# Attention and two feed-forward blocks on one core: a third set of head operands, a second output place, another order of the paired work

## What is computed

```python
# 4 batches, 8 heads, 576 positions, head size 64
scores = (q @ k.T) / 8;  bias = -(cum[i] - cum[j]),  cum = cumsum(max(s, 0))
attn = softmax(where(causal, -1e9, scores + min(bias, 0)))
x = (attn @ v), heads side by side                      # 4 x 576 x 512
h = max(x @ w_in, 0)                                    # 1024 wide
conv = 3 taps along the positions, per channel
x1 = (h * sigmoid(conv)) @ w_out                        # 512 wide
u = x1 + (x1.T @ U @ V).T                               # rank 32, over positions
out = u + max(u @ w_ch1, 0) @ w_ch2                     # 2048 wide
```

## Time and profile before

| | us |
|---|---|
| median of 3 runs | 910.75 (907.56 to 912.88) |
| the profiled execution | 910.62 |
| its span, first to last instruction | 908.8 |
| PE busy in it | 861.6 |
| DVE busy, ACT busy | 468.5, 372.5 |

### The profile page before, as it was taken

The page is one execution under the profiler, slowest core; times in us unless marked ns, Lnnn a source line. Parts: engine busy times, 40 slices in busy tenths (PEclk is TensorE's granted clock), DMA queues, the critical chain, the costliest instruction groups (busy, mean ns, idle before and its releaser), DMA issues.

```text
span 908.8 us, 15655 instructions
## 1 busy us (share of the span) xinstructions
PE 861.6 (95%) x6184; PEld 809.2 (89%) x6184; DVE 468.5 (52%) x984; ACT 372.5 (41%) x709; POOL 50.6 (6%) x105
## 2 busy tenths in 40 slices
PE   4888898989999999999999999999999999999998
PEld 3666888879998999889998999988999999999998
DVE  6788694464445934555344871455323761442222
ACT  2777675554425634544332653444221431221110
POOL 3021000000000000000000000000000000000000
PEclk9999998989999999999999999999999999999999
DMA  7686945636663557336545454435444444274441
GB/s 162 164 228 157 305 141 189 222 73 199 214 209 104 188 167 259 127 106 212 180 152 177 129 172 145 134 100 184 146 145 169 141 174 150 94 240 182 150 175 53
DMA packets 64396, 150.36 MB, mean 165 GB/s; under 512 B 30026, under 2 KB 44362, under 8 KB 51780
## 3 DMA queue, kind: packets, MB, share of 16 engines
q1 hardware_dynamic: 61252, 144.50, 49.4%
q0 software_dynamic: 3072, 4.87, 2.1%
HBM read 119.15 MB, written 30.11 MB: 164 GB/s over the span
## 4 chain that ended last, share of the span: by engine, by line
PE 66%; DVE 13%; issue 10%; ACT 5%; DMA 4%; POOL 1%; SPq 1%; DVEq 0%; ACTq 0%; POOLq 0%
PE psum L1190 18%; PE psum L1192 18%; PE psum L1191 17%; PE psum L1169 5%; DVE work L958 2%; DVE psum L899 2%; PE psum L1116 2%; DVE work L961 2%; DMA few_scratch<-few 2%; PE psum L1148 2%; PE psum L1146 2%; DMA spread_out<-few_scratch 2%; DVE work L956 1%; ACT work L746 1%; DVE ybuf L973 1%
## 5 line engine op out<-in xcount | busy, mean ns | idle before, releaser
L1190 PE MATMUL psum<-r_hl,ring 128*128 128x288 f32 x512 | 153.6, 300 | 3.2 <-DVE r_hl L1001 1.7
L1190 PE MATMUL psum<-uu_hl,ring 128*128 128x288 f32 x512 | 153.2, 299 | 1.5 <-DVE r_hl L1001 1.5
L1192 PE MATMUL psum<-r_hl,ring 128*128 128x288 f32 x512 | 151.2, 295 | 0.0
L1191 PE MATMUL psum<-r_hl,ring 128*128 128x288 f32 x512 | 151.1, 295 | 0.0
L1192 PE MATMUL psum<-uu_hl,ring 128*128 128x288 f32 x512 | 151.0, 295 | 0.0
L1191 PE MATMUL psum<-uu_hl,ring 128*128 128x288 f32 x512 | 150.9, 295 | 0.0
L783 ACT ACTIVATE r_hl<-psum 128x288 fp32r<-128x288 f32 x128 | 52.5, 411 | 188.1 <-PE psum L1192 188.0
L1001 DVE SCALAR_TENSOR_TENSOR r_hl<-psum,r_hl 128x288 fp32r<-128x288 f32 x128 | 58.5, 458 | 134.7 <-ACT r_hl L783 134.6
L1169 PE MATMUL psum<-probs,va 128*65 128x320 f32 (+4 forms) x448 | 109.6, 364 | 6.5 <-ACT probs L694 6.3
L899 DVE CUSTOM_DVE_ANT_0 psum<-psum,key_late 128x512 f32<-128x512 f32 (+4 forms) x160 | 84.9, 564 | 57.1 <-PE psum L1116 56.8
L1190 PEld LDWEIGHTS psum<-r_hl,ring 128*128 128x128 f32 x512 | 96.6, 189 | 5.5 <-DVE u_acc L1013 2.7
(11 more groups left out here) (101 smaller groups left out, 1626.6 us busy)
## 6 DMA issues: line engine op xcount, KB each, us to landing
ring<-w_scratch SPq DMA_DIRECT2D x74, 1024.0 KB, 4.9
w_scratch<-ring SPq DMA_DIRECT2D x24, 1024.0 KB, 6.1
kq_raw<-in_kq_t SPq DMA_DIRECT2D x64, 288.0 KB, 5.0
stage<-in_w_ch SPq DMA_DIRECT2D x16, 512.0 KB, 4.7
spread_out<-few_scratch POOLq DMA_DIRECT2D x32, 144.0 KB, 3.2
out_t<-u_acc SPq DMA_DIRECT2D x16, 288.0 KB, 3.7
va<-in_v SPq DMA_DIRECT2D x32, 128.0 KB, 2.8
stage<-in_w_out SPq DMA_DIRECT2D x4, 512.0 KB, 6.5
```

Of the source, the lines that this page charges most:

```text
L1190: pe.matmul(o, hi, m_hi, start=start, stop=False)
L1191: pe.matmul(o, hi, m_lo, start=False, stop=False)
L1192: return pe.matmul(o, lo, m_hi, start=False, stop=stop)
```

## The change

1. **Third operands.** In body 0, `kb`, `qb`, `qc` get a third buffer (in `r_hl[0]`, not yet in use); the preparation of head n waits for head n-3 and moves from g 3 to g 1 (h < 6), DVE's copies and low parts to g 2. POOL sets one more region to ones.
2. **Two output places.** Heads of batch 0 write by turns to `O0` and `O0 + 4 * BANK`; in body 0 their eviction follows the next head's first exponentials.
3. The weight block's high and low part of body 0 move to g 3; the splits of x pairs 0 and 1 of batch 0 move into the first step of body 1.
4. At (1, 3) the transpose of the maxima moves from g 3 to g 4.
5. In `order`, late pairs stand elsewhere: none between the `gated` items, two behind `wo`, two ahead of `rank`, none behind `split`.
6. `first_products`: at the first `wi`, `wo` and `up` both halves of all tiles but the last are multiplied before the wait for the last tile. `rank` takes the turned tiles in their order and waits for each.
7. In bodies 1 to 3 the low parts of heads come one step later; the eviction follows the step's items where these hold turn, rank or mix; the last inversion of a batch comes at (7, 4) instead of in the next body; other steps for normalisation and splits.
8. For batch 3 the middle tap is on ACT.

```diff
+        def nth_pair(n):
+            return n % 3 if n < H else n % 2
+        def pair_before(n):
+            return max(n - 3, -2) if n < H else n - 2
+        kb, qb, qc = kb + [r_hl[0][:, 0, :]], qb + [r_hl[0][:, 1, :]], qc + [r_hl[0][0:KROWS, 2, :]]
+        def out_at(n):
+            return O0 + 4 * BANK * (n < H and n % 2 == 0)
+        def turn_at(a, h):
+            return TURN[a > 0] + ((a, h) == (1, 3))
             fill(1)
-            seq.append(("gated", b, 0, FT - 1, 0))
-            fill(1)
-            seq.append(("gated", b, 0, FT - 1, 1))
+            seq.extend(pair("gated", b, FT - 1))
             for d in range(KT):
                 seq.extend(pair("wo", b, d))
-            fill(1)
+            fill(2)
...
-                fill(1)
+                fill(2)
                 seq.extend(pair("rank", b, 0))
...
                 seq.append(("split", b, 0, KT - 1, 0))
-                fill(1)
...
-        X_SPLIT = [{(5, 0): 0, (7, 0): 1}, {(4, 0): 0, (6, 0): 1}]
-        X_SPLIT_LAST = [{}, {(0, 2): (NPAIR - 2,), (1, 0): (NPAIR - 1,)}, {(0, 0): (NPAIR - 2,), (0, 2): (NPAIR - 1,)}]
-        NORMALISE = [(4, 6), (3, 5, 7)]
+        EVICT_LATE = {(a, h) for a in PLAN for h in range(H - 1)
+                      if any(x[0] in ("turn", "rank", "mix") for x in PLAN[a][GROUPS * h + GROUPS - 1])}
+        X_SPLIT = {(5, 0): 0, (7, 0): 1}
+        X_SPLIT_LAST = [{}, {(0, 0): (0, 1), (0, 3): (NPAIR - 2,), (1, 0): (NPAIR - 1,)}, {(0, 0): (NPAIR - 2,), (0, 2): (NPAIR - 1,)}]
+        NORMALISE = [{(4, 2): 0, (6, 2): 1}, {(4, 1): 0, (6, 1): 1, (7, 3): 2}]
...
+                pool.memset(qc[2][D:KROWS - 1, :].bitcast(F32), 1.0).then_inc(s_rows1, 1)
...
                 def attention_step(a, h, g):                       # ScalarE
-                    if g == TURN[a > 0]:
+                    if g == turn_at(a, h):
                         max_to_row(a, h + 1)
-                    if g == 3 and not a:
-                        prepare_keys(a, h + 2)
-                        prepare_queries(a, h + 2)
-                    if g == 4:
+                    if g == 4 and (a or h == H - 1) and (a, h) not in EVICT_LATE:
                         evict_head(a, h)
                     for c in {0: (0, 1), 1: (2,), 2: (3,)}.get(g, ()):
                         exponentials(a, h, c)
+                    if g == 0 and h and not a:
+                        evict_head(a, h - 1)
+                    if g == (1 if h < H - 2 else 3) and not a:
+                        prepare_keys(a, h + 2)
+                        prepare_queries(a, h + 2)
...
+                def middle_tap(b, f):
+                    m = b * FT + f
+                    relu.wait(act, b, 2 * f + 2)
+                    yl_done.wait(act, m - 2)
+                    act.activation(conv[f % 2], hid[:, f % 2, 1:S + 1], ACT.Copy, scale=cw[:, 1, f:f + 1]).then_inc(cv.sem, 1)
...
-                    if g == 1 and h in WEIGHTS_HEADS:
+                    if g == 3 and h in WEIGHTS_HEADS:
                         weights_high(MADE[WEIGHTS_HEADS.index(h)])
...
                 def then(a, h, g):                                 # VectorE
-                    if g == 3 and not a:
+                    if g == (2 if h < H - 2 else 3) and not a:
                         highs(a, h + 2)
                         key_low(a, h + 2)
                         query_low(a, h + 2)
-                    if g == 3 and h in (2, 4, 6):
+                    if g == 4 - (a > 0) and h in (2, 4, 6):
                         invert_few(a, h // 2 - 1)
-                    if g == 2 and a:
+                    if g == 3 and a:
                         key_low(a, h + 2)
-                    if g == 3 and a:
+                    if g == 4 and a:
                         query_low(a, h + 2)
+                    if a and (h, g) == (H - 1, 4):
+                        invert_few(a, NPAIR - 1)
...
-                        evict.wait(pe, n - 1)
+                        evict.wait(pe, max(n - 2, -1) if n < H else n - 1)
...
+                def first_products(item, tiles, m_hi, m_lo, ready):
+                    if item[-1] == 0:
+                        other = (*item[:-1], 1)
+                        products(item, tiles, m_hi, m_lo, ready, range(tiles - 1))
+                        if BEFORE[other]:
+                            evicted(BEFORE[other])
+                        products(other, tiles, m_hi, m_lo, None, range(tiles - 1))
+                    return products(item, tiles, m_hi, m_lo, ready, range(tiles - 1, tiles))
```

More of the change, by code:

```diff
@@ L814, in ffn_step @@
                         hidden(b, i, half)
+                        if half and b == B - 1:
+                            middle_tap(b, i)
                         if i and not half:
@@ L926, in then @@
                 def then(a, h, g):
-                    if not a and g == 2 and (h, 0) in X_SPLIT[0]:
-                        x_low(a, X_SPLIT[0][h, 0])
-                    if a and (h, g) in X_SPLIT[1]:
-                        x_low(a, X_SPLIT[1][h, g])
-                    if g == 3 and not a:
+                    if g == (2 if h < H - 2 else 3) and not a:
                         highs(a, h + 2)
@@ L1215, in evicted, with products @@
                         acc.wait(pe, b, NTH[item] + 1)
-                def products(item, tiles, m_hi, m_lo, ready=None):
+                def products(item, tiles, m_hi, m_lo, ready=None, ks=None):
                     half = item[-1]
                     hi, lo = weights(item)
-                    for k in range(tiles):
+                    for k in ks or range(tiles):
                         if ready:
@@ L1230, in wi @@
                     x_ready = lambda k: xl_done.wait(pe, b * NPAIR + k)
-                    products(item, KT, *x_hl, x_ready if f == 0 and half == 0 else None).then_inc(mm_wi.sem, 1)
+                    (products(item, KT, *x_hl) if f else first_products(item, KT, *x_hl, x_ready)).then_inc(mm_wi.sem, 1)
                 def wo(item):
@@ L1235, in wo @@
                     y_ready = lambda k: yl_done.wait(pe, b * FT + k)
-                    products(item, FT, *y_hl, y_ready if d == 0 and half == 0 else None).then_inc(mm_wo.sem, 1)
+                    (products(item, FT, *y_hl) if d else first_products(item, FT, *y_hl, y_ready)).then_inc(mm_wo.sem, 1)
                 def turn(b, t, half):
@@ L1248, in rank @@
                 def rank(b, half):
-                    x1l.wait(pe, b)
                     w = DM // 2
-                    for t in range(NT):
-                        u = [x[:, t, :] for x in u_hl]
-                        m = [x[:, t, half * w:(half + 1) * w] for x in x1t_hl]
-                        mm = three(bank_at("rank", b, 0, 0, half)[:, 0:w], u[0], u[1], m[0], m[1], t == 0, t == NT - 1)
+                    parts = {}
+                    for x in SEQ:
+                        if x[:2] == ("turn", b) and (x[3] < NT - 1 or x[4] == half):
+                            parts[x[3]] = NTH[x] + 1
+                    for x, t in enumerate(sorted(parts, key=parts.get)):
+                        x1l.wait(pe, b, parts[t])
+                        u = [y[:, t, :] for y in u_hl]
+                        m = [y[:, t, half * w:(half + 1) * w] for y in x1t_hl]
+                        mm = three(bank_at("rank", b, 0, 0, half)[:, 0:w], u[0], u[1], m[0], m[1], x == 0, x == NT - 1)
                     mm.then_inc(mm_g.sem, 1)
@@ L1266, in up @@
                     u_ready = lambda k: ul.wait(pe, b, k + 1)
-                    products(item, KT, *uu_hl, u_ready if unit == 0 and f == 0 and half == 0 else None).then_inc(mm_up.sem, 1)
+                    (products(item, KT, *uu_hl) if unit or f else first_products(item, KT, *uu_hl, u_ready)).then_inc(mm_up.sem, 1)
                 def down(item):
```

71 lines of the change are left out of this document (41 added, 30 removed).

## The result

| | before | after |
|---|---|---|
| median | 910.06 us (906.86 to 914.1, 8 runs) | 902.03 us (899.29 to 907.1, 8 runs) |
| ratio | | 0.9912 [0.9883, 0.9942] |
| profiled execution's span | 908.8 us | 901.5 us |

Faster by 0.9%: 8.0 us where 20.0 were forecast, and 2 us above the upper end of the range.

The account below looks back on a forecast made before the run. PE, busy 95% of the span, was taken to be held by VectorE or ScalarE, not weight DMAs. Terms A to G sum to 20.0 us, with 1.7 of hidden waits given back: 910.7 - 20.0 = 890.7, said as 891, range 883 to 900.

Parts of the forecast that it names:

- Term A: Head loop of batch 0 up to the first w_in: shorter PE waits per head, 3.6 us gained, bounds 0 and 7.5.
- the rival of the shared engines: Row sums' spread comes later on the shared DMA engines, 2.0 us at the first w_in: 893, chance 0.08.
- its new wait sets the clock to half: First stage gives nothing, or a new wait at heads 7 and 8 of batch 0 halves the clock: 894.6 to 898, chance 0.17.
- B: Batch 1, head 3, transpose moved to g 4: wait 2.9 and half clock 3.0 go, 5.9 us; bounds 2.4 and 6.3.
- C: Turning, rank and mix of batch 0: waits of 1.50 and 1.20 us go, 2.7 us; bounds 1.2 to 4.
- the fourth rival: Edits move waits instead of removing them, half of terms C to G lost: 896 to 901, chance 0.08.
- The second half-clock stretch: After the mix wait of batch 0; kept in the forecast, costs up to 3.3 us; its going: about 888, chance 0.22.
- D: Batches 1 to 3, waits for x_low before the first w_in: nearly all go, 3.9 us.
- E: Batches 1 to 3, up products' r_hl waits: evictions go behind the items, 1.5 of 3.3 us.
- F: Batches 1 to 3, two r_hl waits of 0.86 at a down soon after its up: both go, 1.7 us.
- G: u_acc wait before batch 3's w_out goes, 0.7 us; the other u_acc waits stay.
- The signs that were named: Batch 0 heads 6.3 to 7.1 us apart, waits gone, PE idle near 30; wrong if new waits over 2 us or half-clock stretches.

Follow-up runs that it names:

- without early blocks: Changed kernel with the two w_out blocks no longer made early in batch 0 but in batch 1: 898.50 us, ratio 0.9897.
- The kernel with the late small load: Kernel before, with the third copy of the taps, U and V loaded at head 5 instead of head 2 of batch 0: 911.89 us, ratio 1.0028.
- without the early stores: Changed kernel without the two 1 MB stores in the stage of batch 0, w_out blocks then holding other numbers: 896.23 us, ratio 0.9871.
- the old loop without early blocks: Changed kernel with no w_out block made early and the head loop of batch 0 as before: 898.88 us, ratio 0.9906.
- The fillers: Idle matmuls ahead of PE's waits in heads 4 to 7 of batch 0, on the changed kernel with small load and store later, three operand pairs to head 11: 900.46 us.

## Why the prediction was wrong

**Term A failed, and with it the number.** "What bounds the stage" was read from the engines: a head of 7.97 us less two waits. The step that failed is "a head free of them is 7.97 - 1.6 = 6.4 us ... 6.8 to 6.9 us a head". It holds for the first heads (6.9 to 7.0 us from mark 2 to mark 4). It leaves out that a faster loop asks sooner for transfers that do not come sooner: the strip of v took 7.9 us to land in the kernel before and 9.6 in the changed one, and the 1.8 us that the old loop had to spare for it became a wait of 3.10. The earlier trace rows had the DMA share at 0.75 over the stage; over 48 to 54 us it was 0.98 in the kernel before, a window that I did not look at. I had the rival of the shared engines, but for the row sums' way before w_in alone, at 2.0 us and a chance of 0.08; in two kernels that way held the maxima inside the stage. The Trainium skill's rule quoted there (page "Trainium Kernel Development and Optimization", Key Constraints, that all queues' transfers share the 16 engines and interleave) agrees with this trace as far as it can show it: POOL's spreads of the row sums landed in a median of 5.3 us between 36 and 64 us, beside SP's loads and stores, and in 3.2 over the whole span. What the runs give for the loop in place of the forecast gain: 5.5 us lost in the profiled stage, 2.7 in the mean of four profiles of the same code, 4.8 in medians with the loop alone on the kernel before, and 2.2 with the rest of the change, which is not clear of noise. (The sum of A also takes the 0.2 us of an inversion off four heads, where the inversions at g 4 of heads 2 and 4 stand ahead of two of them; that is 0.4 us.)

**The other half of A is the clock.** The rival "its new wait sets the clock to half" (0.17, 894.6 to 898) names heads 7 and 8. In the profiled execution half clock came two heads sooner, behind the wait for v, and once more there, so both rivals happened in part, together. The prediction let each cause stand alone. It counted what waits are removed, never what their removal does to the granted clock elsewhere. The runs show that this is of the same size: new loop 5.2 us fewer waits, 4.6 more lost to the clock without early blocks; 0.7 and 5.3 on the kernel before.

**B** was right in place and sized 5.9; it measured 4.8, and 4.6 alone. The wait went; the next late thing, y_low, shows no wait. Of 6.8 us at half clock all went at that place, but in the one kernel with the transpose back only 3.4 had come. The kernel with the late small load had the same 2.87 us wait and no stretch behind it, with marks 12 to 13 at 35.14: the wait alone is 2.1, where the forecast had 2.9 for it, and the 6.8 us at half clock are the other 2.7.

**C** said 2.7 and measured 1.5. Rank's wait went. Mix's went only in name: where one of 1.20 us ended at 195.41, PE now stands for the exponentials (timelines of PE, the changed kernel and the one with no late eviction):

```profile
195.80 1.28 PE L1210 MATMUL psum<-probs,va 128*65 128x320 f32 x2 [1.59 <-ACT probs L717]
...
195.25 1.33 PE L1210 MATMUL psum<-probs,va 128*65 128x320 f32 x2 [1.58 <-ACT probs L717]
```

ScalarE is not ready sooner there in any of the three: an eviction stands ahead of these exponentials, which start at 195.44 us in the kernel before and at 195.31 in the changed one. So 1.2 of the 2.7 us moved instead of going, which the fourth rival describes. Late evictions elsewhere are worth 1.3 us between marks 13 and 14 by the kernel without them. The second half-clock stretch was left in the forecast; of its 6.8 us 3.4 were left in this execution, and none, 3.4, 6.8 or 10.2 in others.

**D, E, F** were right in their sum: 7.0 us in batches 2 and 3. From mark 17 to 25 every kernel that has these edits takes 213.6 us (216.9 before). E alone, by the kernel without late evictions, is 1.1 us in batches 2 and 3, forecast 1.5.

**G and D's end** gave nothing: 1.8 forecast, -0.1 measured. x_hl (1.1) and u_acc (0.7) went, and 1.4 us for y before w_out and 0.6 for uu_hl came, in my reading because an output pair that covered them had moved away; no run puts it back. The forecast's argument that 8.6 us of cover are enough for the 6 us of y's chain did not hold there. Moving the tap to ScalarE did not shorten the chain: VectorE waits for it (timeline of DVE), and PE's wait for y is 1.4 us with the move, 1.2 without:

```profile
717.23 0.82 DVE L1000 SCALAR_TENSOR_TENSOR work<-hid,cw,work 128x576 f32<-128x576 f32 x1 [0.45 <-ACT work L774]
718.09 0.82 DVE L1003 SCALAR_TENSOR_TENSOR work<-hid,cw,work 128x576 f32<-128x576 f32 x1
718.82 0.75 DVE L1015 TENSOR_TENSOR ybuf<-work,ybuf 128x576 fp32r<-128x576 f32 x1
719.66 0.76 DVE L1010 SCALAR_TENSOR_TENSOR work<-work,hid 128x576 f32<-128x576 f32 x1
720.87 0.82 DVE L1000 SCALAR_TENSOR_TENSOR work<-hid,cw,work 128x576 f32<-128x576 f32 x1 [0.45 <-ACT work L774]
```

"Nothing" was right for the tap within 0.2 us.

**The signs that were named.** Heads 1 to 3 came 6.9 to 7.0 us apart, the wait at (1, 3) and the half clock there went, the x_hl and r_hl waits are under 1 us: as forecast. PE's total idle is 901.5 - 861.0 = 40.5 us, not 30, and other half-clock stretches came, which was a sign named for being wrong. The late wait over 2 us was for v, which was not in the list.

**What stays open.** Whether the transfers come late by the load of the 16 engines or by SP, which issues them all in order: between 36 and 54 us it is issuing for 16.3 of 18 us in the changed kernel (15.1 before, 10.4 without the early stores). No kernel takes commands away from SP and leaves the bytes. And why one wait is followed by half clock and another, longer one not. The kernel before waited 1.55 us for exponentials at 92 us with no stretch behind it, the old loop without early blocks 1.5 us at the same place with one. The fillers left the question open too, since the stretch behind the stage grew as those in it went.

## What to carry to other kernels

Before a stage is priced by its engines' waits, list for each transfer in it when it lands and when it is asked for, above all where the DMA share of single windows is near 1 (0.98 here, where the mean was 0.75): the slack between the two, 1.8 us here, is all that a faster loop could gain there before it waited. The share alone does not tell: PE was busy 6.00 of 6 us at 1.09. Without the early blocks, or their stores alone, PE waited for no transfer of the stage in any kernel; moving a load and a store inside it only moved the waits. Where a stage is short of work for PE, count the removal of many small waits and the birth of one larger wait as two different things. And compare stages between marks in the trace rather than medians: here marks 17 to 25 repeat to 0.1 us in all kernels with the same code there, and marks 25 to 32 to 0.3, while executions of one kernel spread over 8 us.

## What the runs showed of the hardware

- The stretches at half clock (1.2 GHz) lasted 3.4, 6.8 or 10.2 us in all 19 profiles, but for up to 2.3 us at the program's very end. Each 3.4 us of it between marks 14 and 17 costs 1.2 to 1.6 us (85.68, 87.30, 88.45, 89.99 us with none to three).
- The same code of batch 0 gave 68.77, 63.09, 66.05 and 66.22 us between marks 1 and 9 in four profiled executions (the changed kernel and those with the transpose, the eviction and the tap put back), with 13.6, 10.2, 13.6 and 13.6 us of it at half clock up to 100 us. The Trainium skill, page "TensorE: Matmul & The Clock Gate", Part 1, says of the slow matmuls at a kernel's start that their number is not fixed: "it's run-variable". The stretches here lie in the middle of a kernel, and by these numbers they vary from execution to execution too.
- Single issues on SP's queue can take long themselves: between 38 and 45 us, at a DMA share of 0.8, one cum_scratch issue took 1.96 us (median 0.25) and one of U 1.83 (0.52 for another of its size; 1.88 for the same one in the kernel before), so SP falls behind without waiting for anyone. What makes them long no run here shows.
